# TensorE's tile loop over all nine turns, with fewer waits, logits in column groups and four late loads, in a fused retention, mixture-of-experts and MLP kernel

## The chip, the cores and the metric

One Trainium2 chip, of which the program uses one core. The metric is the device time of one execution in microseconds (us).

## The reference

Three stages in float32, chained:

```python
# 1: retention over 8 batches, 8 heads, 576 positions, head size 64
scores = np.matmul(q, k.transpose(0, 1, 3, 2)) / np.sqrt(64)
Dmat = np.where(rel >= 0, gamma[:, None, None] ** rel[None], 0.0)   # gamma by head
x = np.matmul(scores * Dmat, v)            # -> x (4608 tokens, 512)
# 2: soft mixture of 8 experts with 4 slots each (32 slots)
logits = x @ phi                           # (4608, 32)
d = softmax(logits, axis=0); slot_input = d.T @ x
slot_out[e] = np.maximum(slot_input[e] @ w1[e], 0) @ w2[e]          # 512 -> 1024 -> 512
c = softmax(logits, axis=1); x = c @ slot_out
# 3: a product of two projections, then two more matmuls
out = (((x @ fw1) * (x @ fw2)) @ w3) @ w_out
```

## The kernel before

The 4608 tokens are 36 tiles of 128, in four groups of nine (a group is two batches). Retention is done in chunks: a chunk of 64 positions takes the running state of its head (64x64, K transposed times V) and adds what lies inside the chunk.

**One tile on TensorE (PE)** has these parts, each a function of the listing. `scores(n+1)` multiplies K and Q in sixteen 64x64 products (each product of two float32 operands is two matmuls in the trace, each with its own weight load); DVE masks them. `update(n+1)` multiplies K and V into the state's increments, which DVE adds up in `next_state` (a ring of eight states). `through_states(n)` sends Q through the states; `through_scores(n, 0)` and, once that half's results are in (`phase_done`), `through_scores(n, 1)` add the masked scores times V. DVE then scales the result into x_t (`scale_x`). Between the two halves stand `turn_x(n-1)` (four 128x128 transposes into the PSUM bank X_NAT, copied by ACT into x_nat) and `logits(n-1)` (x_t as the stationary operand, phi as the moving one, 32 columns). After the last tile of a group `dispatch(g)` (two tiles later) multiplies the exponentials of the group's logits with x_nat; its sums land in X_NAT as well and ACT copies them (`copy_sums`).

**The loop.** Tiles 0 to 3 are written out; a `Fori` over eight turns has a body of four tiles. In it PE waits at the head of each part, with counts computed in registers, and `begin` increments a semaphore of its own behind each wait. Three `If`s in the body hold the dispatches.

**Logits and softmax.** ACT copies each tile's logits (tokens on partitions, slots on the free axis) into logits_raw. Per group, DVE's `max_logits` transposes blocks of 32x32 into exp_t, takes the maxima, ACT takes exponentials in place (`exp_logits`), and DVE transposes back for dispatch (`turn_exp`). `shift_combine` does the other softmax from logits_raw.

**Loads.** SP issues every load in one queue. A tile has K (256 KB), Q (256 KB), and K with V in natural layout (512 KB), in four slots: K waits until the scores of tile n-4 are done, the others until tile n-4 is out (`out_ready`). POOL scales V by its decays (`scale_v`, then `v_ready`). In groups 1 to 3 tiles 0 to 7 are each followed by one load of 512 KB: in turn one of the fold's weights (`load_fold`, 12 in all: w3's two halves and w_out) and half of one expert unit (`load_first_unit`).

**The fold** computes w3 @ w_out with each operand split in a high and a low part (float32r): for each of 16 sets w (two halves of eight), ACT casts w3_hi and wo_hi (`split_hi`), POOL subtracts for w3_lo and wo_lo, and PE does four `fold_part`s of three matmuls. Each of the four buffers has two places, w % 2, so set w waits until set w-2 is used (`fold_used`). The buffers lie over the tile slots and over x_t, so that the first casts wait for the last tile.

**After the loop** PE does turn_x and logits of tile 35, five fold parts, the last dispatch, four parts, the sums of the softmax, two parts, and then 32 expert units (`expert_unit`, 1 MB of weights each) with four or eight fold parts after most groups of four: `fold(4)` after unit 3, `fold(8)` before units 8 and 16 and after 11, 19, 23 and 27. ACT's order is written out: split_hi(0), copies of tile 35's x and logits, the exponentials, split_hi(1) and so on. Eight more units' loads follow as their places come free. The rest (four units, the quadratic features and a loop over nine chunks that gives the output) is not touched.

Constants that the change touches: SLOTS_IN = 4 tile slots, STATES_IN = 8 states, QUARTERS = 4 increments a tile on out_ready and phase_done.

Of the kernel before, what the change touches and what calls it, by code (L numbers as in the profile page):

```python
# [51 lines left out]
STATES_IN = 8  # L52
NAT_RING = 12
QUARTERS = 4

# [22 lines left out]
def build(nc, pkg, consts, phi, units, fold_w, out, c_rows):  # L78
    ctx = ExitStack()
    with ctx:  # L80
# [76 lines left out]
        top[0] = x_at + 62 * KB  # L157

        unit_x = place("unit_x", [P, 3, 2 * FF], at=x_at)  # L160
        wo_lo = place("wo_lo", [P, 2, D], F32R, at=top[1])
        hid_t[0] = place("hid_t0", [P, FT, P], at=top[1])
        unit_y = place("unit_y", [P, 2, 2 * FF], at=top[1])
        w3_hi = place("w3_hi", [P, 2, D], F32R, at=x_at + 50 * KB)
        w3_lo = place("w3_lo", [P, 2, D], F32R, at=top[1])
        wo_hi = place("wo_hi", [P, 2, D], F32R, at=top[1])
        assert top[1] <= top[0], top[1] - top[0]
# [58 lines left out]
        first_v_loaded = sem("first_v_loaded")  # L226
# [3 lines left out]
        fold_loaded = sem("fold_loaded")  # L230
        q_loaded = [sem(f"q_loaded{i}") for i in range(SLOTS_IN)]
# [9 lines left out]
        states_ready = sem("states_ready")  # L241
        last_k_loaded = sem("last_k_loaded")
# [170 lines left out]
        def is_first(n):  # L413

            return isinstance(n, int) and n == 0

# [17 lines left out]
        def _(sp):  # L434
# [20 lines left out]
            def load_fold(g, j):  # L455

                sp.dma_start(fold_raw[:, g - 1, 2 * j:2 * j + 2, :],
                             fold_w[g - 1, j].rearrange("p (j f) -> p j f", j=2)
                             ).then_inc(fold_loaded, 16)
# [11 lines left out]
            def load_k_q(t):  # L471
# [5 lines left out]
            sp.dma_start(pkg_sb[:, 0, 3 * D:4 * D], pkg[0, 2 * P * D:4 * P * D].rearrange(  # L477
                "(p c) -> p c", p=P)[:, D:2 * D]).then_inc(first_v_loaded, 16)
            load_k_q(1)
            sp.dma_start(pkg_sb[:, 0, 2 * D:3 * D], pkg[0, 2 * P * D:4 * P * D].rearrange(  # L480
                "(p c) -> p c", p=P)[:, 0:D]).then_inc(natural_loaded[0], 16)
# [26 lines left out]
            for u in range(6, UNITS):  # L508
# [3 lines left out]
                if u == 9:  # L512

                    sp.wait_ge(logits_ready, NTILES)
# [9 lines left out]
                load_unit(u)  # L524

# [43 lines left out]
        def _(pool):  # L569
            pool.wait_ge(const_loaded, 16)  # L570

            def scale_v(n):
                t = n % TILES
                if n == 0:
                    pool.wait_ge(first_v_loaded, 16)
                else:
                    pool.wait_ge(natural_loaded[place_of(n)], (n // SLOTS_IN + 1) * 16)
# [27 lines left out]
            for w in range(2 * FT):  # L605
# [5 lines left out]
                nc.gpsimd.tensor_tensor(w3_lo[:, w % 2, :], fold_raw[:, half, j, :],  # L611
# [961 lines left out]
```

## Time and profile before

| | |
|---|---|
| median of 3 runs | 429.98 us (429.2 to 430.67) |
| the profiled execution | 429.95 us |
| its span in the profile | 428.2 us |
| mean granted clock of TensorE | 0.952 |
| TensorE busy | 385.6 us, 90% of the span |
| VectorE (DVE), ScalarE (ACT), GpSimd (POOL) busy | 172.1, 120.6, 161.9 us |
| moved by DMA | 104.32 MB, 244 GB/s in the mean |

The time of the profiled execution and its span differ by 1.75 us that lie outside the instructions. Busy times of TensorE come from matmuls that overlap, so a stretch in which it is busy throughout isn't one in which it works at its peak. A granted clock of 1.0 is 2.4 GHz, 0.5 is 1.2 GHz. "Idle before, releaser" names what ended an engine's wait; "issue" means that nothing which the profile shows ended it.

### The profile page before, as it was taken

To read this page: it belongs to the slowest core of one execution; us is meant where nothing else is said; L and a number is where in the kernel's file an instruction comes from. 1 tells how busy PE (TensorE), PEld (TensorE's weight loads), DVE (VectorE), ACT (ScalarE), POOL (GpSimd) and SP (SyncE) were. 2 spreads that over 40 slices of the span, in tenths; PEclk is the share of its full clock that TensorE was granted. 3 is DMA by queue.
4 is the path that set the end of the run, shared out by engine and by line. 5 is a ranking of instruction groups with operands and counts; after the bars stand their busy time and mean duration, and the time that the engine had idled before them with its cause. 6 is when DMAs were issued, how large, how long until landed. Compare 5 with 4: busy or idle time off the path is not lost. (4 is left out here: it accounts for less than half of the span.)

```text
span 428.2 us, 14751 instructions
## 1 busy us (share of the span) xinstructions
PE 385.6 (90%) x6259; PEld 306.4 (72%) x6259; DVE 172.1 (40%) x353; ACT 120.6 (28%) x248; POOL 161.9 (38%) x155
## 2 busy tenths in 40 slices
PE   2697959899999999869988788899999999999997
PEld 2697949698888978856454544446887888888885
DVE  1332415665756466554100400039984333233220
ACT  1010101221222221242122422134264344545442
POOL 1621011112121222036244444218895455554530
PEclk9975668999999999979999999999999999999999
DMA  7853648899999999774988899004723566666322
GB/s 258 311 191 110 218 168 320 297 338 341 376 351 342 344 395 322 244 267 185 417 346 351 334 422 416 8 0 84 211 99 121 175 209 218 209 215 209 129 98 100
DMA packets 38191, 104.32 MB, mean 244 GB/s; under 512 B 4052, under 2 KB 6676, under 8 KB 34324
## 3 DMA queue, kind: packets, MB, share of 16 engines
q1 hardware_dynamic: 38164, 103.95, 67.5%
q8 instruction: 18, 0.29, 0.3%
q14 instruction: 9, 0.07, 0.0%
HBM read 93.62 MB, written 10.32 MB: 243 GB/s over the span
## 5 line engine op out<-in xcount | busy, mean ns | idle before, releaser
L581 POOL TENSOR_TENSOR pkg_sb<-pkg_sb,const_sb 128x512 f32<-128x512 f32 x36 | 37.6, 1044 | 133.4 <-DMA pkg_sb<-in_tiles 133.4
L637 POOL TENSOR_TENSOR feat<-c_sb 128x512 f32<-128x512 f32 x45 | 56.8, 1273 | 46.2 <-PE psum L1029 44.3
L1029 PE MATMUL psum<-m_hi,feat_hi 128*128 128x512 f32 x144 | 56.1, 390 | 0.2 <-DVE m_lo L1470 0.2
L1029 PE MATMUL psum<-m_hi,feat_lo 128*128 128x512 f32 x144 | 56.0, 389 | 0.0
L1029 PE MATMUL psum<-m_lo,feat_hi 128*128 128x512 f32 x144 | 56.0, 389 | 0.0
L1045 ACT COPY x_nat<-psum 128x512 f32<-128x512 f32 x36 | 21.0, 584 | 119.8 <-PE psum L747 119.8
L1253 DVE TENSOR_TENSOR x_t<-psum,x_decay 128x512 f32<-128x512 f32 x36 | 24.8, 688 | 74.4 <-PE psum L731 74.4
L424 DVE TENSOR_TENSOR feat_lo<-feat,feat_hi 128x512 fp32r<-128x512 f32 x34 | 27.3, 802 | 62.1 <-ACT feat_hi L1160 61.0
L611 POOL TENSOR_TENSOR w_lo<-fold_raw,w_hi 128x512 fp32r<-128x512 f32 x16 | 20.6, 1287 | 58.5 <-ACT wo_hi L1093 58.5
L731 PE MATMUL psum<-weights_t,pkg_sb 64*64 64x64 f32 x1152 | 35.9, 239 | 5.5 <-issue 5.3
L1160 ACT CAST feat_hi<-feat 128x512 fp32r<-128x512 f32 x45 | 27.9, 622 | 39.4 <-POOL feat L637 39.4
L833 PE MATMUL psum<-wo_hi,w_hi 128*128 128x512 f32 x64 | 27.9, 436 | 11.7 <-POOL wo_lo L613 5.4
L759 PEld LDWEIGHTS psum<-phi_sb,x_t 128*128 128x128 f32 x288 | 38.4, 207 | 0.0
L759 PE MATMUL psum<-phi_sb,x_t 128*128 128x32 f32 x288 | 38.2, 279 | 0.0
L675 PE MATMUL psum<-pkg_sb 64*64 64x64 f32 x1152 | 28.1, 240 | 9.4 <-DMA pkg_sb<-in_tiles 4.3
L731 PEld LDWEIGHTS psum<-weights_t,pkg_sb 64*64 64x64 f32 x1152 | 27.3, 147 | 7.4 <-issue 5.6
L694 PE MATMUL psum<-pkg_sb 64*64 64x64 f32 x1152 | 27.8, 239 | 5.2 <-DMA pkg_sb<-in_tiles 3.5
L675 PEld LDWEIGHTS psum<-pkg_sb 64*64 64x64 f32 x1152 | 24.4, 152 | 11.3 <-issue 6.6
L1029 PEld LDWEIGHTS psum<-m_hi,feat_hi 128*128 128x128 f32 x144 | 27.0, 188 | 6.2 <-issue 0.6
L715 PE MATMUL psum<-pkg_sb,state_sb 64*64 64x64 f32 x1152 | 27.9, 238 | 4.0 <-issue 2.0
L1029 PEld LDWEIGHTS psum<-m_hi,feat_lo 128*128 128x128 f32 x144 | 27.0, 188 | 5.6
L1029 PEld LDWEIGHTS psum<-m_lo,feat_hi 128*128 128x128 f32 x144 | 27.0, 188 | 5.6
(125 smaller groups left out, 583.2 us busy)
## 6 DMA issues: line engine op xcount, KB each, us to landing
pkg_sb<-in_tiles SPq DMA_DIRECT2D x78, 256.0 KB, 5.1
pkg_sb<-in_tiles SPq DMA_DIRECT2D x31, 512.0 KB, 5.2
c_sb<-c_rows SPq DMA_DIRECT2D x45, 256.0 KB
unit_a<-in_units SPq DMA_DIRECT2D x10, 1024.0 KB, 10.9
unit_x<-in_units SPq DMA_DIRECT2D x9, 1024.0 KB, 9.3
out<-out_sb SPq DMA_DIRECT2D x36, 256.0 KB, 2.1
fold_raw<-in_fold SPq DMA_DIRECT2D x12, 512.0 KB, 5.8
unit_a<-in_units SPq DMA_DIRECT2D x12, 512.0 KB, 6.4
```

The lines of the kernel that those rows point to most:

```text
L424: engine.tensor_tensor(feat_lo[:, k, :], feat[:, k, :], feat_hi[:, k, :].bitcast(F32), ALU.subtract).then_inc(done, 1)
L581: nc.gpsimd.tensor_tensor(v_nat(n).rearrange("p (h d) -> p h d", h=HEADS), v_nat(n).rearrange("p (h d) -> p h d", h=HEADS), decay.unsqueez ...
L637: nc.gpsimd.tensor_tensor(feat[:, k, :], c_sb[:, s, x, :], c_sb[:, s, y, :], ALU.mult).then_inc(feat_ready, 1)
L675: last = mm(psum[cols, odd, HD * a:HD * (a + 1)], k_t(r)[rows, a, cols], q_t(r)[rows, a, cols], start=True, stop=True)
L694: last = mm(psum[HD * odd:HD * (odd + 1), UPDATE + half, HD * a:HD * (a + 1)], k_nat(r)[rows, cols], v_nat(r)[rows, cols], start=True, sto ...
L715: mm(out_of(a, odd, half), state_sb[rows, 2 * r + half, a, :], q_t(r)[rows, a, HD * half:HD * (half + 1)], start=(half == 0 and a < 2), st ...
L731: last = mm(out_of(a, odd, half), v_nat(r)[rows, HD * h:HD * (h + 1)], weights_t[rows, r % 2, odd, HD * a:HD * (a + 1)], start=False, stop ...
L759: last = mm(psum[:, RAW, 0:SLOTS], x_t[:, r % 2, a, :], phi_sb[:, a, :], start=(a == 0), stop=(a == PAIRS - 1))
L833: last = mm(psum[:, f, :], a[:, w % 2, P * f:P * (f + 1)], b[:, w % 2, :], start=(j == 0 and m == 0), stop=(j == FT - 1 and m == 2))
L1029: last = mm(psum[:, OUT + b, :], x, y, start=(at == 0 and m == 0), stop=(at == 4 and m == 2))
L1160: copy(feat_hi[:, ORDER[at], :], feat[:, ORDER[at], :]).then_inc(feat_hi_ready, 1)
L1253: tt(x_t[:, n % 2, :, :].rearrange("p (k b) n -> p k (b n)", k=2), psum[:, OUT_T:OUT_T + 2, 0:D // 2], x_decay[:, :, n0:n0 + P].rearrange( ...
```

## The change

1. **Loop.** The four tiles written out are gone: the `Fori` has nine turns. To make the counts fit, ACT increments `x_nat_ready` and `logits_copied` by NAT_AHEAD = 2 beforehand, and the parts of a tile that don't exist in the first or the last turn stand in an `If`.
2. **Waits.** PE waits at two points of a tile: before `turn_x` (x_t, the copies of two tiles ago), and before the second half of through_scores, for everything that the next tile's scores and update need: K, Q and scaled V of tile n+2, the masks of tile n+1, its states. `turn_x(n-1)` moves ahead of `through_states(n)`; a dispatch moves behind the logits.
3. **States.** The ring has four states in place of eight; DVE waits for `states_used`, which through_states increments after its first half.
4. **Logits.** phi is the stationary operand (32 columns) and x_t the moving one, in four column groups of 32 tokens. The result has slots on partitions, so the block transposes are of no use to max_logits and exp_logits, which read logits_raw; shift_combine gets one instead.
5. **Fold.** The two places of the four buffers are separate tiles; place 0 overlaps nothing of the tile loop, so split_hi(0) waits for its loads alone. After the loop stand fold(2), turn_x, logits, fold(4), dispatch, fold(4), then fold(2) before the experts (12 parts in place of 11).
6. **Loads.** w3's first half comes in group 1, w_out in group 2, nothing of the fold in group 3; w3's second half (four loads) behind expert units 12 to 15. Tile 0's natural K and V are one load, ahead of tile 1's K and Q.

```diff
-STATES_IN = 8
+STATES_IN = 4
+NAT_AHEAD = 2
...
+        fold_hl = [{}, {}]
+        for n in ("w3_hi", "wo_hi", "w3_lo", "wo_lo"):
+            fold_hl[0][n] = place(n + "0", [P, D], F32R)
...
-                        if t % 2 == 0:
-                            load_fold(g, t // 2)
-                        else:
+                        if t % 2 == 0 and g < 3:
+                            load_fold(2 * g - 1, t // 2)
+                        elif t % 2:
                             load_first_unit(g, t // 4, t // 2 % 2)
...
                 load_unit(u)
+                if 12 <= u < 16:
+                    load_fold(2, u - 12)
...
             def logits(r):
                 for a in range(PAIRS):
-                    last = mm(psum[:, RAW, 0:SLOTS], x_t[:, r % 2, a, :], phi_sb[:, a, :],
-                              start=(a == 0), stop=(a == PAIRS - 1))
-                last.then_inc(logits_ready, 1)
+                    for j in range(SUBS):
+                        last = mm(psum[SLOTS * j:SLOTS * (j + 1), RAW, 0:SLOTS], phi_sb[:, a, :],
+                                  x_t[:, r % 2, a, SLOTS * j:SLOTS * (j + 1)],
+                                  start=(a == 0), stop=(a == PAIRS - 1))
...
             def step(i, r):
                 n = i * SLOTS_IN + r
...
+                if r < SLOTS_IN - 1:
+                    scores(ahead[1])
+                    update(ahead[1])
...
+                def turn():
+                    pe.wait_ge(x_t_ready, n)
+                    pe.wait_ge(x_nat_ready, n - 1 + NAT_AHEAD)
+                    pe.wait_ge(logits_copied, n - 1 + NAT_AHEAD)
+                    pe.sem_inc(tile_begun, 1)
+                    turn_x(before)
...
+                through_states(r)
+                through_scores(r, 0)
+                if r > 0:
+                    logits(before)
...
+                            dispatch(g)
+                pe.wait_ge(phase_done, n * QUARTERS + QUARTERS)
+                if r < SLOTS_IN - 2:
+                    next_loaded(i, r)
+                    next_free(n)
+                    pe.sem_inc(tile_begun, 1)
...
+                through_scores(r, 1)
+
+            def next_loaded(i, r):
+                turn, place = divmod(r + 2, SLOTS_IN)
+                pe.wait_ge(k_loaded[place], i * 16 + (turn + 1) * 16)
+                pe.wait_ge(q_loaded[place], i * 16 + (turn + 1) * 16)
+                pe.wait_ge(v_ready, i * SLOTS_IN + (r + 3))
+
+            def next_free(n):
+                pe.wait_ge(masked, n + 2)
+                pe.wait_ge(states_ready, n * 2 + 5)
...
+            with pe.Fori(0, NTILES // SLOTS_IN) as i:
                 for r in range(SLOTS_IN):
                     step(i, r)
...
-            turn_x(NTILES - 1, SLOTS_IN - 1)
-            logits(NTILES - 1, SLOTS_IN - 1)
-
             pe.wait_ge(masked, NTILES)
+            fold(2)
+
             pe.wait_ge(x_t_ready, NTILES)
-            fold(5)
+            pe.wait_ge(x_nat_ready, NTILES - 1 + NAT_AHEAD)
+            turn_x(SLOTS_IN - 1)
+            pe.wait_ge(logits_copied, NTILES - 1 + NAT_AHEAD)
+            logits(SLOTS_IN - 1)
+
+            fold(4)
...
             def split_hi(w):
                 half, j = divmod(w, FT)
                 if w == 0:
-                    act.wait_ge(fold_loaded, 16 * 12)
+                    act.wait_ge(fold_loaded, 16 * 8)
+                if w >= FT and w % 2 == 0:
+                    act.wait_ge(fold_late_loaded[(w - FT) // 2], 16)
+                if w == 1:
                     act.wait_ge(out_ready, QUARTERS * NTILES)
-                    act.wait_ge(x_t_ready, NTILES)
+                    act.wait_ge(logits_ready, SUBS * NTILES)
...
             def next_state(c):
+                if c >= 3 and c % 2 == 1:
+                    dve.wait_ge(states_used, QUARTERS * ((c - 3) // 2 + 1))
...
             def max_logits(g):
-                if g > 0:
-                    dve.wait_ge(exp_nat_ready, g)
-                nc.vector.transpose(exp_t[:, :], logits_raw[:, g % 2, :]).then_inc(raw_turned, 1)
-                dve.wait_ge(raw_turned, g + 1)
-                nc.vector.tensor_reduce(neg_part[:, :], exp_t[:, :], AX.X, ALU.max, negate=True).then_inc(part_max, 1)
+                nc.vector.tensor_reduce(neg_part[:, :], logits_raw[:, g % 2, :], AX.X, ALU.max, negate=True).then_inc(part_max, 1)
```

## Rows read from the trace of the kernel before

**Rows 1.** Busy times by stretch: us, then busy (count) by engine, PEclk, DMA share, GB/s.

```profile
0.00:41.50 41.50, 27.30 (x756) 25.60 (x760) 11.79 (x23) 4.37 (x9) 12.55 (x16) 0.82 0.66 224
41.50:91.40 49.90, 43.65 (x1294) 39.59 (x1291) 22.02 (x50) 8.30 (x22) 8.35 (x8) 0.81 0.73 255
91.40:129.90 38.50, 37.15 (x1297) 33.01 (x1289) 23.30 (x54) 8.29 (x22) 9.40 (x9) 1.00 0.97 351
129.90:168.80 38.90, 37.00 (x1288) 32.87 (x1289) 23.74 (x55) 8.30 (x22) 9.40 (x9) 1.00 0.98 351
168.80:184.30 15.50, 14.30 (x496) 13.17 (x496) 8.19 (x17) 3.09 (x8) 2.09 (x2) 1.00 0.81 280
184.30:202.80 18.50, 14.76 (x88) 10.38 (x89) 10.33 (x26) 5.89 (x14) 9.65 (x8) 0.82 0.54 201
202.80:284.30 81.50, 72.70 (x456) 40.08 (x459) 7.59 (x16) 20.55 (x39) 31.33 (x25) 1.00 0.74 304
```

**Rows 2.** Timeline of PE over one tile: start, length, engine, line, operation, count.

```profile
103.64 0.65 PE L675 MATMUL psum<-pkg_sb 64*64 64x64 f32 x32
104.27 0.69 PE L694 MATMUL psum<-pkg_sb 64*64 64x64 f32 x32
104.90 0.69 PE L715 MATMUL psum<-pkg_sb,state_sb 64*64 64x64 f32 x32
105.39 0.44 PE L731 MATMUL psum<-weights_t,pkg_sb 64*64 64x64 f32 x16
105.76 0.65 PE L747 MATMUL psum<-const_sb,x_t 128*128 128x128 f32 x4
106.25 0.98 PE L759 MATMUL psum<-phi_sb,x_t 128*128 128x32 f32 x8
107.16 0.46 PE L731 MATMUL psum<-weights_t,pkg_sb 64*64 64x64 f32 x16
107.44 0.65 PE L675 MATMUL psum<-pkg_sb 64*64 64x64 f32 x32
```

**Rows 3.** The same timeline where a group is broken in two.

```profile
18.35 0.33 PE L675 MATMUL psum<-pkg_sb 64*64 64x64 f32 x3 [2.07 <-issue]
...
59.44 0.49 PE L731 MATMUL psum<-weights_t,pkg_sb 64*64 64x64 f32 x7 [4.64 <-issue]
```

**Rows 4.** DMA queues of instructions, of 12 to 62 and of 62 to 200 us.

```profile
q8 instruction: 10, 0.16, 1.7%
...
q14 instruction: 4, 0.03, 0.1%
```

**Rows 5.** Busy times of one stretch at the low clock.

```profile
37.30:50.40 13.10, 13.04 (x299) 12.66 (x302) 4.06 (x8) 1.55 (x4) 2.09 (x2) 0.51 0.34 99
```

**Rows 6.** Timeline of PE, the second part of the first dispatch.

```profile
80.12 0.40 PE L778 MATMUL psum<-x_nat,exp_nat 128*32 128x128 f32 x8
```

**Rows 7.** Natural K and V loads (L448) of 84 to 180 us, issue to landing.

```profile
DMA to landing us min/median/max: 3.5/4.9/6.4
```

**Rows 8.** Page, part 2: what the DMA moved in each fortieth.

```profile
GB/s 258 311 191 110 218 168 320 297 338 341 376 351 342 344 395 322 244 267 185 417 346 351 334 422 416 8 0 84 211 99 121 175 209 218 209 215 209 129 98 100
```

**Rows 9.** Timeline of the seam: first casts and what they release.

```profile
185.23 0.62 ACT L1092 CAST w_hi<-fold_raw 128x512 fp32r<-128x512 f32 x1 [1.11 <-DVE x_t L1253]
...
189.08 0.76 PE L833 MATMUL psum<-wo_hi,w_hi 128*128 128x512 f32 x1 [2.43 <-POOL wo_lo L613]
...
190.28 0.61 ACT L1092 CAST w_hi<-fold_raw 128x512 fp32r<-128x512 f32 x1
...
194.59 0.47 PE L833 MATMUL psum<-wo_hi,w_hi 128*128 128x512 f32 x1 [0.43 <-POOL wo_lo L613]
```

**Rows 10.** PE's waits between the experts (203 to 284 us): total, times, longest.

```profile
PE psum L833 <- ACT wo_hi L1093: 4.7, 4, 1.2
PE psum L833 <- POOL wo_lo L613: 2.6, 2, 1.4
PE psum L833 <- DVE w_lo L1334: 1.5, 1, 1.5
```

More of the change, by code:

```diff
@@ L230, in build @@
         fold_loaded = sem("fold_loaded")
+        fold_late_loaded = [sem(f"fold_late_loaded{j}") for j in range(FT // 2)]
         q_loaded = [sem(f"q_loaded{i}") for i in range(SLOTS_IN)]
@@ L782, in step @@
                 n = i * SLOTS_IN + r
-                turn, following = divmod(r + 1, SLOTS_IN)
-                here = [g for g in range(GROUPS - 1) if dispatched_at(g) % SLOTS_IN == r]
-                def ahead():
-                    scores(n + 1, following, (i + (turn + 1)) * 16)
-                    update(n + 1, following)
-                if isinstance(i, int) or r < SLOTS_IN - 1:
-                    ahead()
+                before = (r + SLOTS_IN - 1) % SLOTS_IN
+                ahead = [(r + m) % SLOTS_IN for m in range(3)]
@@ L792, in step @@
+                if r < SLOTS_IN - 1:
+                    scores(ahead[1])
+                    update(ahead[1])
                 else:
                     with pe.If(i < NTILES // SLOTS_IN - 1):
-                        ahead()
-                if not isinstance(i, int):
-                    for g in here:
+                        scores(ahead[1])
+                        update(ahead[1])
+                def turn():
[4 more added lines that the diff above has]
+                    turn_x(before)
@@ L797, in step @@
+                if r > 0:
+                    turn()
+                else:
+                    with pe.If(i > 0):
+                        turn()
+                through_states(r)
+                through_scores(r, 0)
+                if r > 0:
+                    logits(before)
+                else:
+                    with pe.If(i > 0):
+                        logits(before)
+                for g in range(GROUPS - 1):
+                    if dispatched_at(g) % SLOTS_IN == r:
                         with pe.If(i == dispatched_at(g) // SLOTS_IN):
@@ L798, in step @@
                             dispatch(g)
-                through_states(n, r)
-                through_scores(n, r, 0)
-                if not is_first(n):
-                    if not isinstance(i, int):
-                        for g in here:
-                            with pe.If(i == dispatched_at(g) // SLOTS_IN):
-                                pe.wait_ge(sums_copied, g + 1)
-                                pe.sem_inc(tile_begun, 1)
-                    before = (r + SLOTS_IN - 1) % SLOTS_IN
-                    turn_x(n - 1, before)
-                    logits(n - 1, before)
@@ L811, in step @@
-                through_scores(n, r, 1)
-            scores(0, 0, 16)
-            update(0, 0)
-            for r in range(SLOTS_IN):
-                step(0, r)
-            with pe.Fori(1, NTILES // SLOTS_IN) as i:
+                pe.wait_ge(phase_done, n * QUARTERS + QUARTERS)
[3 more added lines that the diff above has]
+                    pe.sem_inc(tile_begun, 1)
+                else:
+                    with pe.If(i < NTILES // SLOTS_IN - 1):
+                        next_loaded(i, r)
+                        pe.sem_inc(tile_begun, 1)
+                    if r == SLOTS_IN - 2:
+                        next_free(n)
+                        pe.sem_inc(tile_begun, 1)
+                    else:
+                        with pe.If(i < NTILES // SLOTS_IN - 1):
+                            next_free(n)
+                            pe.sem_inc(tile_begun, 1)
```

146 lines of the change are left out of this document (63 added, 83 removed).

## The prediction

> **What bounds the kernel now.** I read the busy times by stretch first, cutting the span where the work changes [rows 1]. The last 143.9 us (428.2 less the first seven rows) hold nothing that the change edits, so its price lies in the first 284.3 us. There, 91.4 to 168.8 is eighteen tiles with TensorE busy 37.15 of 38.5 and 37.00 of 38.9 us, but with the DMA engines at a share of 0.97 and 0.98 too: both are at their end. The two stretches before are worse for the same work (41.5 to 91.4 is nine tiles as well, and takes 49.9), at a granted clock of 0.81 to 0.82, with the DMA idle for a quarter to a third. 202.8 to 284.3 (experts with the fold between) has TensorE idle for 8.8 us and DMA at 0.74.
>
> Second, the timeline of TensorE over one undisturbed tile [rows 2]: 3.80 us from scores to scores. Scores take 0.63, the update 0.63, states 0.49, first half of through_scores 0.37, turn_x 0.49, logits 0.91, second half 0.28. Third, the places where a group of matmuls is broken in two by idle time that nothing releases [rows 3]: 2.07 us in the third scores, 4.64 us in the last tile of the loop's first turn. The DMA view [rows 4] shows what stands beside them: ten 16 KB instruction loads on q8 between 12 and 62 us and none between 62 and 200, while the loop's body repeats seven times. So a piece of code costs at its first pass, and the kernel has eight tiles of first pass (four written out, four of the body). After such a gap the clock is at its lower level, 1.2 GHz: 37.3 to 50.4 ran at 0.51, and its 299 matmuls are 2.14 tiles (140 each in rows 2), 6.1 us a tile instead of 3.8 [rows 5].
>
> Last I read the seam (184.3 to 202.8) in time order, and the waits between the experts.
>
> **Tiles, TensorE's side.** Logits: eight matmuls 114 ns apart become 32 of 32 moving columns on 32 output rows. Rows 2 has sixteen 64-column matmuls in four quadrants in 0.28 us, 70 ns for four. Half the columns puts four between 35 and 70 ns, so eight fours take 0.28 to 0.56; I take 0.45. The nearest row of the new shape is L778, eight of 128 columns in 0.40 with the last one's tail [rows 6], 50 ns each, so 1.6 us is the upper end. The turn moves ahead of states, one more change between whole-array and quadrant work: 0.09 (0.37 less 0.28). Waits go from seven points to two: scores and update take 0.63 where states, the same 32 matmuls, take 0.49, so up to 0.28 goes; I take 0.15. Tile: 3.80 - 0.91 + 0.45 + 0.09 - 0.15 = 3.3 us (3.0 to 5.0).
> New waits: the state ring of four makes DVE's next_state wait for through_states of the same tile, with mask and scale_x queued behind it; both are needed only a scores-and-update (1.3 us) later, so I cost this at 0, up to 0.3 a tile. K, Q and V of tile n+2 are now waited for before the second half of tile n, about 0.9 us earlier than update(n+2) needed V. The V load takes 3.5 to 6.4 us to land, 4.9 in the median [rows 7], and is issued when tile n-2 is out; two tiles of 3.8 make 7.6 us, from which 0.5 of issue, 1.0 of POOL and 0.3 of the second half leave 5.8. The slowest loads will stall PE, most will not. Cost 0 while DMA bounds anyway.
>
> **Tiles, DMA's side.** Nine tiles with both extra loads moved 13.5 MB (351 GB/s over 38.5 us) at share 0.97. That is 37.3 us of pure DMA, so a quicker tile brings at most 1.2 us there. The low end: best slices of the page reach 416 to 422 GB/s [rows 8], 32.5 us. In the third such stretch four loads of 512 KB leave: 2.1 MB of 13.65, 5.9 of 38.1 us, leaving 32.2; PE needs 9 x 3.3 + 2.1 for a dispatch = 31.8.
> By stretch:
> - 0 to 41.5: the first stall stays (same code up to there). The loop then reads its code once; four tiles at the low clock partly. One of the two later stalls (about 2 us) and its low-clock tile (2.3) go, tiles are 0.4 shorter: -6.0. Bounds -10.5 and 0. The one load of K and V for tile 0 in place of two is within 1 us either way.
> - 41.5 to 91.4: stall of 4.64 and two spells of low clock go; what is left is the DMA's 37.3: 38.0, -11.9 (34 to 46).
> - 91.4 to 129.9: 37.5, -1.0 (33 to 40).
> - 129.9 to 168.8: 32.8, -6.1 (31 to 38.9).
> - 168.8 to 184.3: four tiles at 3.3 and the wait for x_t: 14.3, -1.2 (13 to 16).
>
> **The seam.** Before, TensorE turned the last tile, and the fold began 3.85 us after ACT's first cast (185.23 to 189.08) because POOL's two low parts come between [rows 9]. Now fold(2) stands ahead of turn_x and logits. ACT reaches split_hi(0) only after copy_logits(34), whose logits end about 0.4 us before the last tile. So fold weights come at 3.6 us after the tile loop, PE has nothing else, the clock falls, two fold parts take 2.6 us (0.43 a matmul at that level) and the last logits end at about 7.4, where before it was 2.4. From there: copy and maxima 2.4 (0.5 less, no transpose), exp to the second cast 0.7, and 4.3 from that cast to PE (190.28 to 194.59 [rows 9]) less 0.4: 14.2. fold(4) takes two parts before and two after that, the latter at the low clock 2.6, then dispatch about 3, fold(4) 2.8, slot_in and fold(2) 2.4: 25.0 against 18.5, +6.5. If the first two parts were ready in time it would be +0.5.
>
> **Experts.** Parts before unit 0 go from 5+4+2 = 11 to 2+4+4+2 = 12. Four parts use one weight set and two sets fit. With eleven, each block of eight parts reaches into a third set, which PE waits for: 4.7 + 2.6 + 1.5 = 8.8 us [rows 10]. With twelve each block ends with its set, and the next two are cast while PE does four units (3.6 us against 3.9). -8.8, and -0.7 for the part already done: 72.0. Upper end 81.5. The moved loads are 2.1 MB, about 5 us at the 0.42 MB/us of the best slices [rows 8]. Now the stretch has 0.26 x 81.5 = 21 us of DMA free and its last unit lands well ahead; in 72 us with 5 more 7 are left. They stand in SP's queue ahead of units 13 to 16, used over 20 us later. Cost 0; without that cover 5.
>
> **Sum**, on the profiled execution (span 428.2, time 429.95, equal to the median 429.98): -6.0 -11.9 -1.0 -6.1 -1.2 +6.5 -9.5 = -29.2, span 399.0, time 401.
>
> **Rivals.**
> A, quicker: the DMA gives its better rate once loads are asked for sooner (33.5 in each of two nine-tile stretches, -8.5), or the seam costs only 0.5 (-6). One of them: 393 to 395; both 387. For: slices at 420. Against: share 0.97 with 351 GB/s. 0.15.
> B, the start keeps its stalls: the body's tile has 328 instead of 280 TensorE instructions, so the first pass meets the same waits for code, only earlier, and the early V wait adds bubbles. -6.0 becomes 0 and -11.9 becomes -6: 413. 0.15.
> C, column groups don't overlap: logits 1.6, tile 4.6, nine tiles 43.5 and four 19.5. Against my stretches +5.5, +6, +10.7 and +5.2: 428, no change. 0.03.
> D, the slower side: the body stops staying resident. From rows 2 and the dispatches (72 x 2 instructions) it was 4 x 280 + 144 = 1264 and becomes 4 x 328 + 144 = 1456 besides waits. If its head has been dropped at the back edge, each of eight turns meets a gap as in rows 3 (4.64), and about 3 us of low clock after it: 7.6 x 8 = 61, less some DMA slack, about 450. It decides from 3.7 us a turn. For: ten loads in the first pass show that code is big against what is kept. Against: seven repeats without a load. 0.08.
> The Trainium skill (Runtime: NRT & Kernel Launch, "Instruction fetch mechanics") gives TensorE 2048 instructions in 16 KB blocks, and says a branch out of a two-page window stalls. The quiet 62 to 200 us disagree with the second and agree with the first, by which a body of 1456 and some hundred waits just fits.
>
> **Chances.** Forecast 0.58, its own range 396 to 407; A 0.15, B 0.15, C 0.03, D 0.08, and 0.01 for no visible effect. Range 387 to 416: below it hardly anything, above it C and D. Within 0.3% (what a measurement here tells from none): 0.02; slower 0.09; faster 0.89.
>
> **What would show it.** Instruction loads on q8 end about 20 us earlier and none recur in the loop (D: they do, every turn). Scores to scores near 3.8 us and DMA at 0.97 or more in the loop's second and third group, 3.5 in the last. L833 starts 3.5 us after the last tile, ahead of the last turn. No idle before L833 between units. Logits under 0.6 us. Wrong if the nine-tile stretches fall below 34 or stay at 38.9 after the fold's loads have gone, or if the seam stays under 20.

## The result, and the profile after

The changed kernel takes **423.37 us** (median of 4 runs, 421.77 to 424.58) against 430.0 for the kernel before on the same chip: ratio 0.984, 95% interval [0.980, 0.989]. The forecast was 401 with a range of 387 to 416: the direction was right and the size was not. The profiled execution took 424.19 us with a span of 422.4, against 428.2 before. Medians and spreads below are of all runs of a kernel; a ratio leaves out a run that is over 1.5% above the fastest of the same kernel, which here is one of experiment 10 (418.4 us) and two of the kernel before beside experiments 5 to 8.

First the busy times by stretch, with the same columns and cut at the same events as [rows 1] (scores of tiles 6, 15, 24 and 33, the end of the last tile, the first expert unit); the last row ends with the experts.

```profile
0.00:43.70 43.70, 22.92 (x849) 20.19 (x853) 11.79 (x23) 4.37 (x9) 12.29 (x16) 0.96 0.62 213
43.70:82.80 39.10, 31.91 (x1514) 26.62 (x1508) 21.60 (x50) 8.18 (x22) 8.60 (x9) 1.00 0.92 321
82.80:124.30 41.50, 33.37 (x1516) 27.89 (x1509) 22.97 (x54) 8.18 (x22) 9.38 (x9) 0.96 0.92 325
124.30:166.50 42.20, 33.54 (x1513) 27.95 (x1505) 22.88 (x54) 8.18 (x22) 9.77 (x10) 0.96 0.82 286
166.50:182.70 16.20, 12.36 (x592) 10.50 (x592) 7.89 (x17) 3.81 (x10) 1.70 (x2) 1.00 0.73 250
182.70:208.30 25.60, 17.42 (x115) 11.50 (x114) 9.82 (x26) 5.10 (x12) 10.68 (x8) 0.73 0.38 144
208.30:277.00 68.70, 68.70 (x439) 39.52 (x438) 7.21 (x15) 19.20 (x35) 30.66 (x25) 1.00 0.95 392
```

| stretch | before | forecast | after | off by |
|---|---|---|---|---|
| to step 5 | 41.5 | -6.0 | 43.7 (+2.2) | +8.2 |
| steps 5 to 13 | 49.9 | -11.9 | 39.1 (-10.8) | +1.1 |
| steps 14 to 22 | 38.5 | -1.0 | 41.5 (+3.0) | +4.0 |
| steps 23 to 31 | 38.9 | -6.1 | 42.2 (+3.3) | +9.4 |
| steps 32 to 35 | 15.5 | -1.2 | 16.2 (+0.7) | +1.9 |
| seam | 18.5 | +6.5 | 25.6 (+7.1) | +0.6 |
| experts | 79.9 | -9.5 | 68.7 (-11.2) | -1.7 |
| the rest | 145.5 | 0 | 145.4 (-0.1) | -0.1 |

(The row of before for the experts, 81.5, ended 1.6 us later, at 284.3; both kernels are cut here at the first matmul after the experts.) The last column sums to 23.4 us, which is the whole miss (-5.8 against -29.2). The five rows of tiles alone are off by 24.6. The experts and the seam came as forecast.

One undisturbed tile of the changed kernel, PE alone, as [rows 2]:

```profile
139.03 0.46 PE L693 MATMUL psum<-weights_t,pkg_sb 64*64 64x64 f32 x16 [0.66 <-issue]
139.29 0.68 PE L655 MATMUL psum<-pkg_sb 64*64 64x64 f32 x32
139.75 0.68 PE L666 MATMUL psum<-pkg_sb 64*64 64x64 f32 x32
140.45 0.63 PE L701 MATMUL psum<-const_sb,x_t 128*128 128x128 f32 x4
141.01 0.69 PE L681 MATMUL psum<-pkg_sb,state_sb 64*64 64x64 f32 x32
141.52 0.41 PE L693 MATMUL psum<-weights_t,pkg_sb 64*64 64x64 f32 x16
141.87 0.46 PE L707 MATMUL psum<-x_t,phi_sb 128*32 128x32 f32 x32
142.92 0.29 PE L693 MATMUL psum<-weights_t,pkg_sb 64*64 64x64 f32 x4 [0.60 <-issue]
```

From start to start it is 3.89 us, longer than the 3.80 of before, though the logits (L707) went from 0.91 to 0.46 us. Take away the idle 0.60 that lies between the two starts and 3.29 are left: the matmuls do cost what was forecast (3.3). The idle time is new and stands where the block of waits is, ahead of the second half of `through_scores`. Other tiles wait longer, as PE's waits from step 5 to the last tile show (line waiting, releaser, total, times, longest):

```profile
PE psum L693 <- issue: 12.3, 17, 1.1
PE psum L693 <- DVE state_sb L1251: 7.0, 5, 2.0
PE psum L693 <- POOL pkg_sb L574: 4.3, 3, 2.0
PE psum L693 <- DVE state_sb L1247: 2.0, 3, 0.7
```

That is 25.6 us in front of one line (L693), 16.0 of them in the eighteen tiles of steps 14 to 31; the kernel before had 2.1 in front of all its lines together in those steps. L574 is `scale_v`, L1251 and L1247 are `next_state`. The waits between the experts are gone, as forecast: the view lists none there, where [rows 10] had 8.8 us. And the code is read once, as was said. These are queue 8's instruction loads of 12 to 62 us, six beside ten in [rows 4]; the next one comes at 190 us, behind the loop:

```profile
q8 instruction: 6, 0.10, 0.8%
```

The seam in order of time: the fold starts 3.0 us after the last tile, then the turn and the logits of tile 35, then parts that wait 5.17 us for POOL, then the dispatch, as the prediction had it.

```profile
185.71 0.77 PE L830 MATMUL psum<-wo_hi,w_hi 128*128 128x512 f32 x1 [3.01 <-POOL wo_lo L606]
...
188.41 1.06 PE L701 MATMUL psum<-const_sb,x_t 128*128 128x128 f32 x4
...
197.47 0.77 PE L830 MATMUL psum<-wo_hi,w_hi 128*128 128x512 f32 x1 [5.17 <-POOL wo_lo L606]
...
200.30 2.58 PE L723 MATMUL psum<-x_nat,exp_nat 128*32 128x512 f32 x16
```

### The profile page after: what moved, and what is told of

Same layout as the page of the kernel before. It is cut to its first block and busy times, and to the rows that moved or that the text cites. A ratio compares the mean times of both kernels' runs of the same rounds, so it can differ in the third digit from the quotient of the medians.

```text
span 422.4 us, 16426 instructions
## 1 busy us (share of the span) xinstructions
PE 360.4 (85%) x7123; PEld 276.4 (65%) x7123; DVE 170.1 (40%) x353; ACT 120.2 (28%) x248; POOL 162.2 (38%) x155
## 5 line engine op out<-in xcount | busy, mean ns | idle before, releaser
L574 POOL TENSOR_TENSOR pkg_sb<-pkg_sb,const_sb 128x512 f32<-128x512 f32 x36 | 37.5, 1042 | 130.3 <-DMA pkg_sb<-in_tiles 130.3
L693 PE MATMUL psum<-weights_t,pkg_sb 64*64 64x64 f32 x1152 | 32.8, 229 | 35.5 <-issue 21.5
L693 PEld LDWEIGHTS psum<-weights_t,pkg_sb 64*64 64x64 f32 x1152 | 25.6, 139 | 39.0 <-issue 39.0
L655 PE MATMUL psum<-pkg_sb 64*64 64x64 f32 x1152 | 27.0, 233 | 8.3 <-DMA pkg_sb<-in_tiles 4.4
L666 PE MATMUL psum<-pkg_sb 64*64 64x64 f32 x1152 | 27.0, 234 | 3.0 <-POOL pkg_sb L574 3.0
L655 PEld LDWEIGHTS psum<-pkg_sb 64*64 64x64 f32 x1152 | 23.4, 147 | 9.3 <-issue 4.8
L1251 DVE TENSOR_TENSOR state_sb<-psum,state_sb 128x256 f32<-128x256 f32 x56 | 23.6, 421 | 12.4 <-PE psum L681 10.3
L1215 ACT COPY out_sb<-psum 128x512 f32<-128x512 f32 x36 | 21.1, 587 | 21.5 <-PE psum L1030 19.5
L1229 DVE TENSOR_TENSOR weights_t<-psum,const_sb 128x512 f32<-128x512 f32 x36 | 24.6, 683 | 5.6 <-PE psum L655 5.4
```

Source lines behind the costliest of these rows:

```text
L574: nc.gpsimd.tensor_tensor(v_nat(n).rearrange("p (h d) -> p h d", h=HEADS), v_nat(n).rearrange("p (h d) -> p h d", h=HEADS), decay.unsqueez ...
L655: last = mm(psum[cols, odd, HD * a:HD * (a + 1)], k_t(r)[rows, a, cols], q_t(r)[rows, a, cols], start=True, stop=True)
L666: last = mm(psum[HD * odd:HD * (odd + 1), UPDATE + half, HD * a:HD * (a + 1)], k_nat(r)[rows, cols], v_nat(r)[rows, cols], start=True, sto ...
L693: last = mm(out_of(a, odd, half), v_nat(r)[rows, HD * h:HD * (h + 1)], weights_t[rows, r % 2, odd, HD * a:HD * (a + 1)], start=False, stop ...
L1229: tt(weights_t[:, n % 2, :, :].rearrange("p k (a n) -> p k a n", a=PAIRS), psum[:, 0:2, 0:D // 2].rearrange("p k (a n) -> p k a n", a=PAIR ...
L1251: tt(to, new, state_sb[:, c % STATES_IN, :, :].rearrange("p a n -> p (a n)"), ALU.add).then_inc(states_ready, 1)
```

## The experiments

"T" is the end of the last tile in the profiled execution: 184.3 before, 182.7 after. It is a figure of one execution, and experiments 7 and 12, whose tile loops are the same, differ by 6.6 us in it, 6.4 of them before step 14; their steps 14 to 31 take 71.9 and 71.7 us. So steps 14 to 31 are the firmer measure: 77.4 us before, 83.7 after. Ratios are to the kernel before, on the same chip; experiments 1 to 4, 5 to 8 and 9 to 12 ran on three different chips.

**1. Fewer waits in the block.** K's and Q's waits move to POOL, ahead of `scale_v`; two that others imply are dropped.

```diff
+                pool.wait_ge(k_loaded[place_of(n)], (n // SLOTS_IN + 1) * 16)
+                pool.wait_ge(q_loaded[place_of(n)], (n // SLOTS_IN + 1) * 16)
-                pe.wait_ge(k_loaded[place], ...); pe.wait_ge(q_loaded[place], ...)
-                pe.wait_ge(masked, n + 2)
-                pe.wait_ge(x_nat_ready, n - 1 + NAT_AHEAD)
```

> The changed kernel, with three of the waits by a register's value fewer at the point before the second half of through_scores (K and Q are waited for by POOL ahead of its scaling of V, so v_ready stands for them; states_ready stands for the masks, since DVE makes them in order) and one fewer before turn_x. Nothing computed changes. Theory S (TensorE's sequencer needs about 0.1 us for each register operation or wait, and begins with them only when the matmuls ahead of them are nearly all issued; the trace of the changed kernel has seven of them over 0.85 us between the last logits matmul and the next one): about three sequencer instructions go, the idle 0.60 to 0.66 us before that half becomes 0.3 to 0.4, the commonest step falls from 3.9 to 3.6 us, 423.4 becomes 412 to 416. Theory W (the half waits for data: DVE's state sum that the four-state ring holds back, or V): the idle stays 0.6, the time stays within 2 us of 423. Theory D (DMA bounds the tiles): shorter idle in single tiles, but nine-tile stretches stay at 41 to 42 us.

420.06 us (418.44 to 424.17), ratio 0.974 [0.967, 0.981], T 182.1. In the profile nothing is gained: nine tiles still take 41.8 and 41.1 us. The short idle times did shrink, from some 0.66 to 0.40 us, as theory S had it. But the waits for POOL grew to 11.2 us in eight places, where the changed kernel had 4.3 in three.

**2. The logits' matmuls done twice.** This was meant to put work into the idle time. What it showed is what a longer body costs.

```diff
+                for again in range(2):
                     for a in range(PAIRS):
```

> The changed kernel, with each tile's 32 logits matmuls done twice into the same place (the second pass starts the sum anew, so the result is the same). About 0.2 to 0.25 us more of TensorE work stands between through_scores' first half and the waits. Theory S: the waits begin only after the added matmuls, the idle stays about 0.6 us and each step grows by 0.2 to 0.25 us: 35 steps, 7 to 9 us, 431. Theory W (data not there yet): the added work fills the idle, which falls to 0.35 to 0.4, steps and time stay (423 plus or minus 2). Theory D: the same as W.

602.13 us (one run), T 360.6. On the three theories it says nothing, since something else overran them all. Nine tiles take 93.6 us. PE executes 1618 instructions a turn instead of 1362, and queue 8 makes 79 instruction loads up to 360 us, some nine in each turn, where the changed kernel makes 6 up to its last tile, all before 38 us:

```profile
q8 instruction: 79, 1.29, 1.5%
```

This is rival D, alive one step further on; the change itself stays short of it.

**3. The turn and the logits of tile 35 ahead of the fold.**

```diff
-            fold(2)
             pe.wait_ge(x_t_ready, NTILES)
...
             logits(SLOTS_IN - 1)
-            fold(4)
+            fold(6)
```

> The changed kernel, with turn_x and logits of the last tile ahead of the fold again and six fold parts after them, before the dispatch (in place of two before and four after). The prediction's reason for the seam (fold(2) holds the last logits back for 3 us until POOL's low parts are there, and the clock falls twice): the seam of 25.6 us falls to 19 to 21, the time to 417 to 419. Rival (the seam is set by the sum of TensorE's work and the second weight set, whatever comes first): within 1.5 us of 423.

416.45 us (415.0 to 419.54), ratio 0.967 [0.959, 0.976]. T is 182.1, about as after, and the seam is back at 18.3 us, where before had 18.5. So its price was `fold(2)` in front of the turn.

```profile
182.10:200.40 18.30, 15.36 (x117) 10.44 (x114) 9.86 (x26) 5.09 (x12) 10.31 (x8) 0.81 0.53 198
```

**4. The kernel before with the column-group logits alone.**

```diff
-                    last = mm(psum[:, RAW, 0:SLOTS], x_t[:, r % 2, a, :], phi_sb[:, a, :], ...
+                    for j in range(SUBS):
+                        last = mm(psum[SLOTS * j:SLOTS * (j + 1), RAW, 0:SLOTS], phi_sb[:, a, :],
+                                  x_t[:, r % 2, a, SLOTS * j:SLOTS * (j + 1)], ...
```

> The kernel before with the logits in four column groups alone (and with it the transposes moved from the maxima to the other softmax). Everything else as before, seven wait points a tile included. Theory S: logits take 0.3 to 0.35 in place of 0.91 us and the waits behind them (three sequencer instructions at most at any point) show about 0.15 us more: steps of 3.80 become 3.3 to 3.4. Where DMA bounds (theory D, the prediction's step), the nine-tile stretches fall only from 38.5 and 38.9 to 37.3 or a little more; if it doesn't, they fall to 34 to 35. So D: 425 to 427; not D: 414 to 418.

419.57 us (416.37 to 419.86), ratio 0.971 [0.963, 0.979]: one part alone gains no less than all of them together, though it stays 1.6 us above the 418 expected. Steps 14 to 22 and 23 to 31:

```profile
88.90:125.20 36.30, 33.69 (x1516) 28.04 (x1508) 23.30 (x54) 7.80 (x25) 9.51 (x10) 1.00 1.01 377
125.20:160.30 35.10, 33.29 (x1508) 27.56 (x1500) 23.23 (x55) 7.97 (x24) 9.39 (x9) 1.00 1.04 388
```

The DMA moves 377 and 388 GB/s with all loads in their old place, where [rows 1] had 351 at a share of 0.97. So 37.3 us is no floor, and the tiles of the changed kernel (325 and 286 GB/s) are held by something of its own.

**5. The block of waits behind the second half,** with one increment more.

```diff
                 pe.wait_ge(phase_done, n * QUARTERS + QUARTERS)
-                ... the block ...
+                pe.sem_inc(tile_begun, 1)
                 through_scores(r, 1)
+                ... the block ...
```

> The changed kernel with the block of waits for the next two tiles (K, Q, V, masked scores, states) moved from in front of the second half of through_scores to behind it, so that out_ready(n) no longer stands behind V(n+2) and state(2n+4). Same number of waits. Theory V (the wait for V(n+2) and the states ahead of out(n) closes a loop through POOL, DVE and SP's load and makes long waits): the waits of 0.7 to 2.0 us under L574, L1251 and L1247 (13.3 us between 41 and 182) mostly go, nine tiles take 38 to 39 instead of 41.5 us, the last tile ends at 174 to 177 instead of 182.7, the kernel takes 415 to 418 us. Theory S (what costs is the 0.1 us that PE's queue needs for each register instruction of that block, some 0.6 us a tile, wherever it stands): nine tiles still take 41 to 42 us, the last tile ends at 181 to 184, the kernel takes 422 to 424 us; the idle time only changes its line from through_scores to scores.

419.61 us (417.66 to 420.86), ratio 0.972 [0.963, 0.982], T 178.1, nine tiles 40.4 and 39.7. Between the two theories: the waits put down to POOL and DVE fall from 13.3 to 5.0 us, and idle time that nothing releases now stands in front of `scores` (10.8 us in 18 places).

**6. Both 1 and 5.**

> The same move, and the block cut to its V and state waits (K and Q waited for by POOL ahead of scale_v, masked and x_nat waits left to what implies them). V and S together: both the long waits and most of the 0.6 us go, nine tiles take 34 to 36 us, the last tile ends at 166 to 171, the kernel takes 406 to 411 us. V alone: as waits_after_half, 415 to 418. S alone: as few_waits before it (nine tiles 41, 420 us).

413.84 us (413.17 to 416.58), ratio 0.961 [0.951, 0.971], T 172.3, nine tiles 38.1 and 38.0. The cut block that gained nothing in 1 gains 5.8 us of T here. So both costs are real, and in 1 the early wait had taken up what the shorter block freed. It is still 1.3 us short of the 171 at most that the two theories together allowed.

**7. The waits at seven points again,** each in front of its group and for the tile that it needs; the loop over nine turns, order, logits and loads as in the changed kernel.

```diff
+                    pe.wait_ge(k_loaded[place], ...); pe.wait_ge(q_loaded[place], ...)
+                    pe.wait_ge(masked, n + 1)
                     scores(ahead[1])
+                    pe.wait_ge(states_ready, n * 2 + 3)
+                    pe.wait_ge(v_ready, n + 2)
                     update(ahead[1])
...
-                ... the block ahead of through_scores(r, 1) ...
```

> The changed kernel with the waits spread again over seven points of a tile, each in front of the group of matmuls that needs it and for tile n+1 alone, the loop over all nine turns, its order of groups, column-group logits and the late fold loads kept. PE's queue then handles more register instructions in a turn than the changed kernel (50). Theory V: nothing waits early, nine tiles take 35 to 37 us as with the logits change alone, the last tile ends at 172 to 176, the kernel takes 411 to 416 us. Theory S in its plain form (time goes with the number of register instructions in PE's queue): nine tiles take 42 to 44 us, the last tile ends at 184 to 188, the kernel takes 424 to 428 us. A third, W (the instructions cost only where they stand in one clump, since the queue runs a few of them ahead of the matmuls): as V, but with gaps of 0.1 to 0.2 us at each of the seven points instead of one of 0.6.

406.53 us (404.44 to 408.01), ratio 0.941 [0.931, 0.950], T 167.1. This is the largest single step of the study, and T is 5 us below what even theory V allowed. PE's queue handles 63 register instructions a turn instead of 50 and T falls by 15.6 us (steps 14 to 31 from 83.7 to 71.9): the plain count was the wrong theory. A tile and steps 14 to 31:

```profile
128.04 0.46 PE L693 MATMUL psum<-weights_t,pkg_sb 64*64 64x64 f32 x16 [0.20 <-issue]
128.37 0.69 PE L655 MATMUL psum<-pkg_sb 64*64 64x64 f32 x32
128.89 0.69 PE L666 MATMUL psum<-pkg_sb 64*64 64x64 f32 x32
129.52 0.66 PE L701 MATMUL psum<-const_sb,x_t 128*128 128x128 f32 x4
130.10 0.69 PE L681 MATMUL psum<-pkg_sb,state_sb 64*64 64x64 f32 x32
130.62 0.41 PE L693 MATMUL psum<-weights_t,pkg_sb 64*64 64x64 f32 x16
130.96 0.46 PE L707 MATMUL psum<-x_t,phi_sb 128*32 128x32 f32 x32
131.35 0.46 PE L693 MATMUL psum<-weights_t,pkg_sb 64*64 64x64 f32 x16
```

```profile
80.90:117.10 36.20, 33.44 (x1515) 27.95 (x1504) 22.77 (x54) 8.13 (x23) 9.40 (x9) 1.00 1.01 378
117.10:152.70 35.60, 33.02 (x1500) 27.61 (x1500) 23.09 (x55) 8.42 (x23) 9.51 (x9) 1.00 0.94 332
```

3.31 us from start to start: the forecast tile, with seven points of waiting instead of two. It is one of the quicker ones; the tile before it took 3.57. In it the seven groups flow into one another with no idle time at their waits, but for 0.20 at L693. Over all tiles from step 5 on, 4.0 us stand there in 20 places, and 2.9 in seven in front of `scores`.

**8. The late loads put back** into the third group of tiles.

```diff
-                        if t % 2 == 0 and g < 3:
-                            load_fold(2 * g - 1, t // 2)
+                        if t % 2 == 0:
+                            load_fold((1, 3, 2)[g - 1], t // 2)
```

> The changed kernel with the third of the fold's weights (w3's second half, four loads of 0.5 MB) loaded in the third group of tiles again instead of among the experts. Theory D' (the DMA traffic bounds the tiles of that stretch, as the prediction's 6.1 us for steps 23 to 31 had it): that stretch takes 46 to 48 us instead of 42.2, the kernel takes 428 to 430 us. Theory V or S (PE's own waits bound it): 42 to 43 us, the experts stay at 68.7 us, the kernel takes 423 to 425 us.

425.11 us (420.56 to 426.8), ratio 0.982 [0.971, 0.993] against 0.984 for the changed kernel: no difference that shows. Steps 23 to 31 take 42.3 us with the loads and 42.2 without, at 324 GB/s instead of 286. Moving 2.1 MB out of that stretch brought nothing, because DMA didn't bound it. (Steps 14 to 22, where nothing was moved, took 43.7 us here instead of 41.5: so much can lie between two executions of the changed kernel's tiles.)

**9 to 11. What the block costs, taken apart.** Each adds one thing to 7, in front of `through_scores(r, 1)`: as many register waits, increments and branches in the source as the changed kernel has there, but for counts long reached (9); the wait for V(n+2) alone (10); the wait for the state behind update(n+1) alone (11).

```diff
                 pe.wait_ge(phase_done, n * QUARTERS + QUARTERS)
+  9:            pe.wait_ge(k_loaded[r], ...); pe.wait_ge(q_loaded[r], ...); pe.wait_ge(v_ready, n + 1)
+                pe.wait_ge(masked, n + 1); pe.wait_ge(states_ready, n * 2 + 2); ...
+ 10:            pe.wait_ge(v_ready, n + 3)
+ 11:            pe.wait_ge(states_ready, n * 2 + 5)
```

> seven_points with the changed kernel's block of waits put back in front of the second half of through_scores in its instructions alone: five more register waits and one or two more increments, with the same branches in the third and fourth tile of a turn, but for what tile n has long had (its own K, Q, V, masked scores and state), so that nothing is ever waited for. Last tile of seven_points: 167.1, of the changed kernel 182.7. Theory W (a clump of instructions in PE's queue costs because the queue runs only a little ahead of the matmuls): about 0.3 to 0.5 us a tile over 35 tiles, the last tile ends at 177 to 184 us, the kernel takes 417 to 423 us, with an idle time of 0.5 to 0.7 us in front of L-through_scores in every tile. Theory V (what costs is what the block waits for): 167 to 169 us, the kernel takes 406 to 409 us.

> seven_points with one wait more in front of the second half of through_scores: for V of tile n+2, as the changed kernel has it there. Theory V (that wait makes out(n), and with it the load into the slot that comes free, stand behind the load and scaling of V(n+2)): long waits on POOL come back, the last tile ends at 173 to 181 us instead of 167.1, the kernel takes 412 to 420 us. Theory W: one instruction more of 0.1 us, mostly hidden, the last tile ends at 167 to 170 us, the kernel takes 406 to 409 us. The branches of the third and fourth tile add two to three instructions there.

> seven_points with one wait more in front of the second half of through_scores: for the state behind update(n+1) (states_ready at 2n+5), as the changed kernel has it there. DVE makes that state after the masked scores of tile n+1 and after x_t(n-1) and what belongs to a group's end. Theory V in its second form (the DVE row of the changed kernel, 7.0 and 2.0 us between 41 and 182, is this wait): the last tile ends at 171 to 177 us instead of 167.1, the kernel takes 411 to 416 us. Theory W: 167 to 169, the kernel takes 406 to 409 us.

| | time | ratio | T | steps 14 to 31 |
|---|---|---|---|---|
| the changed kernel | 423.37 | 0.984 [0.980, 0.989] | 182.7 | 83.7 |
| 7 | 406.53 | 0.941 [0.931, 0.950] | 167.1 | 71.9 |
| 9, instructions alone | 412.55 (411.75 to 415.02) | 0.960 [0.954, 0.967] | 171.2 | 76.8 |
| 10, early V | 414.08 (410.84 to 418.4) | 0.959 [0.950, 0.967] | 171.4 | 76.9 |
| 11, early state | 414.36 (412.96 to 416.97) | 0.965 [0.958, 0.971] | 171.2 | 77.2 |

The largest waits at L693 in each, from step 5 to the last tile, for 7, 9, 10 and 11 in turn (9 has 3.4 us more in seven places, put down to DVE and POOL, though it awaits nothing that is late; 11 has 1.4 in three):

```profile
PE psum L693 <- issue: 4.0, 20, 0.2
```

```profile
PE psum L693 <- issue: 9.6, 21, 0.7
```

```profile
PE psum L693 <- POOL pkg_sb L574: 10.0, 12, 1.5
PE psum L693 <- issue: 5.2, 16, 0.6
```

```profile
PE psum L693 <- DVE state_sb L1255: 7.3, 6, 1.6
PE psum L693 <- issue: 5.6, 14, 0.6
```

Every theory was half right, and each expected its rival's experiment to show nothing. Steps 14 to 31 grow by 4.9 us with the clump (a block of instructions that waits for nothing), by 5.0 with early V and by 5.3 with the early state (T by 4.1, 4.3 and 4.1; for the clump its own theory had 10 and more). Together that is 15.2 us, more than the 11.8 by which the changed kernel is slower there than 7. So the costs overlap and don't add up, and no share of the whole can be given to each.

Nor are the three clean of one another. The trace shows PE's register instructions, and one instruction can do two of the source's waits. From the last logits matmul to the second half of `through_scores` it has 7 of them a turn in experiment 7, 18 in 9, 15 in 10, 13 in 11 and 30 in the changed kernel. So 9 added 11, less than half of what the change added, and 10 and 11 carry 8 and 6 more of their own. What speaks for the early waits beside that is the length of single ones: up to 1.5 and 1.6 us, where their instructions alone make 0.3 to 0.6.

Where nothing is late and no dispatch lies between, the idle time there goes with the number of instructions: 0.20 us for two (7), 0.30 for three (10), 0.42 for four and 0.71 for six (9), 0.61 to 0.66 for six, 0.70 for seven and 1.09 for ten (the changed kernel). Only the third tile of a turn has some 0.1 less (0.33 for four, 0.60 for seven). By the smallest values of each of a turn's tiles, some 20 of the changed kernel's 25.6 us at L693 are the block itself and 5 to 6 what it waits for. That is an estimate of the idle time, not of the gain: experiment 1 shortened the block and gained nothing while the early waits stood.

**12. Experiment 7 with experiment 3's seam.**

> seven_points with the turn of x(35) and its logits ahead of the fold's first six parts, as in seam_turn_first. If the two add up: the last tile ends at 167 us, then 18.3 us to the first expert matmul instead of 25.0, experts 68.7, rest 145.4, a span of 399 to 400 us and a time of 399 to 401 us. If the earlier end of the tiles leaves something else late there (the first twelve parts need the splits on ACT and POOL, which then start earlier too): 20 to 22 us in that place, 402 to 404 us.

**396.58 us** (394.77 to 399.0), ratio 0.922 [0.916, 0.929], the fastest of all: below both kernels, and 6.3% below the changed one by the ratios (0.922 / 0.984). T 160.5, seam 19.6, experts 68.7. That is 2.4 us below the 399 that it was expected to take at best. The shorter start (38.7 us to step 5 instead of 42.4, and 35.8 for the next nine instead of 38.5) comes from nothing that this edit touches. It may be luck or the other chip, though all four runs are within 399.0 us; against it, the seam is 19.6, not 18.3.

## Why the prediction was wrong

**The step that failed** is the tile's waits, which the forecast had at a gain. It was put in three sentences: waits "from seven points to two ... I take 0.15" saved; K, Q and V of tile n+2 awaited early at "Cost 0 while DMA bounds anyway"; and the state ring at 0, up to 0.3. The saving was a loss: 25.6 us of idle time at the second point, steps 14 to 31 at 83.7 us where 70.3 was forecast, and 71.9 with the seven points back (experiment 7). The prediction read the gap between 0.63 for scores or update and 0.49 for states as the price of waiting. But scores and update together take 1.15 us from start to start in experiment 7, behind waits that are met, and 1.16 in the changed kernel, without any. A wait met in time costs nothing that shows as long as PE has matmuls in hand. Gathered in one place the instructions stand open. In the tile of 139.03 us the last logits matmul has begun when six register instructions follow, 0.10 to 0.14 us apart from 138.37 to 138.93, and the next matmul after them; experiment 7's tile has two there. That is 0.66 us idle against 0.20, or some 0.11 for each of four more, and experiment 9 shows it with nothing awaited (0.42 for four).

**The cushion for V** was worked out with the wrong tile. 5.8 us against a median landing of 4.9 [rows 7] took two tiles of 3.8; with the forecast's own 3.3 it is 2 x 3.3 - 1.8 = 4.8, less than the median. At the pace of its forecast stretches (37.5 us for nine tiles) it would be 6.5, but wherever PE ran at its own pace, V would be late about half the time. Nor does "DMA bounds anyway" cover it, since in the listing `out_ready` stands behind the wait and is what releases the next loads into the slot. So an early wait there can make slack for DMA instead of using it. That fits the shares: in steps 14 to 22, with the same loads, it was 0.97 before, 0.92 in the changed kernel and 1.01 in experiment 7 (351, 325 and 378 GB/s). No run shows the single load that was issued late for it. The state wait is the same case through DVE, and the prediction didn't name it among the early ones; the longest at L1251 is 2.04 us.

**Point by point.** *To step 5* (+8.2 off): rival B's first half. The first turn reads as much code as before, six loads on queue 8 up to step 5 in both kernels. PE's waits at L693 without a releaser are 9.2 us there (five times, longest 3.7), where before had 4.8 at all lines. What is gone are the four loads and the 4.6 us of the next stretch. What each of the 9.2 us waited for isn't shown; the block takes its 0.6 to 1.1 a tile here too. *Steps 5 to 13*: the number is right (39.1 for 38.0), at a granted clock of 1.00 instead of 0.81, and the stall of 4.6 is gone as forecast. What holds the rest is not the forecast's: the DMA share is 0.92, and 6.8 us stand idle at L693. So the closeness is partly luck. Here the loop over all nine turns pays: in experiment 4, which keeps four tiles written out, the stretch takes 47.2, in experiment 7 it takes 38.5. *Steps 14 to 31*: the failed step; the part of it that rested on the late loads (-6.1) was void, as experiment 8 shows, and experiment 4 takes 35.1 us for steps 23 to 31 with these loads in their old place. Nor does any run reach the 32.8 forecast there: 7 and 12 take 35.6 and 36.2, with PE busy for 33.0 and 33.2, where the forecast had 31.8 for all of PE's work. *DMA's floor* of 37.3 was too high by 1 to 2 us: the rate rose to 377 to 388 GB/s when PE asked sooner (experiments 4 and 7). A share of 0.97 did not mean that the rate was spent. This was rival A's mechanism, and it decided nothing in the changed kernel. *Logits*: 0.46 with the tail and about 0.4 from start to start, for 0.45 forecast; rival C is out. *Seam*: 25.6 for 25.0, by the mechanism given (experiment 3). *Experts*: no wait left, as worked out; -11.2 for -9.5. *Rival D*: not here, but its mechanism is real (experiment 2).

*Where a body stops fitting.* On this the Trainium skill (Runtime: NRT & Kernel Launch, "Instruction fetch mechanics") has 2048 instructions of room and a stall at a branch out of two pages. No turn of the changed loop, 1362 instructions executed (1411 with a dispatch) and a branch back over all of them, loaded anything after the first; at 1618 each one loaded some nine times. So the trace disagrees with the second figure, and the point where a body stops fitting lies below the first: between 1435 (the longest turn of any kernel here that stayed resident, experiment 9's with a dispatch) and 1618 executed, to which the dispatches that are stepped over (about 49 instructions each, two or three of them) have to be added.

## What to carry to other kernels

Put a wait in front of the work that needs it, however many waits that makes; many met waits among busy matmuls cost less than a few gathered or early ones. When a cost is taken apart one cause at a time, check that the parts don't sum to more than the whole, and count in the trace what an edit really put in. Before a wait is moved ahead of a signal, ask what that signal releases: here it releases the next loads, and the wait closes a loop through SP, POOL and DVE. Work out a cushion with the period that you forecast, not with the one that you measured.

## What the hardware showed

- About 0.1 us for each register instruction in TensorE's queue where no matmuls cover it (0.20 us idle for two, 0.42 for four, 0.61 to 0.71 for six), and nothing that shows where they do (experiments 7 and 9, the changed kernel). Two of the source's waits can be one such instruction.
- 32 matmuls of 32 columns in four column groups start within 0.4 us at the full clock, each with a weight load of 0.11 us of its own, where eight of the other orientation took 0.91.
- A DMA share of 0.97 at 351 GB/s in one kernel and of 1.01 at 378 in another, with the same loads of the same sizes: the share alone doesn't say that the rate is at its end.
- A body that outgrows what is kept costs much more than one pass of its code: 93.6 us instead of 39.1 for nine tiles, 602 us in all.
